# Three moves in a spectral mixture-of-experts kernel: folds on one engine, spectrum columns in halves, the first row list inside the limit search

## The reference, cut to what matters

```
X = np.fft.fft(np.fft.fft(x, axis=1), axis=2).real          # x: 4 x 2496 x 256, float32
x = X.reshape(9984, 256)
# first mixture, 8 experts of 1024 hidden units
logits = x @ w_gate                                          # 9984 x 8
# all (token, expert) pairs in falling order of logit; a token goes to the first expert
# with room left, each expert takes 9984/8 = 1248 tokens
out[assigned to e] = np.maximum(x @ w1[e], 0) @ w2[e]
# second mixture: expert = argmax of its own gate, no capacity
y = softmax_top * sigmoid(x @ w_output_gate)[e] * (relu(x @ w1[e]) @ w2[e])
```

## Time and profile before

| | value |
|---|---|
| median of 3 executions | 1362.06 us |
| the profiled execution: its own time | 1359.75 us |
| its span, first to last instruction | 1358.0 us |
| mean granted TensorE clock | 0.935 |
| PE busy | 1278.2 us (94%) |
| DVE busy | 764.1 us (56%) |
| POOL busy | 571.4 us (42%) |
| ACT busy | 324.8 us (24%) |
| transform: first to last table matmul | 10.81 to 95.6 us |
| features | 95.6 to 133.7 us |
| first five phases | 135.8 to 254.6 us |
| first list | to 289.1 us |
| first product of the first mixture | 298.66 us |

### The profile page before, as it was taken

How to read it: one execution, slowest core, us unless ns; L and a number is a source line. 1 busy time by engine, 2 the same in 40 slices (tenths; PEclk the granted TensorE clock), 3 DMA queues, 4 the chain that set the end, 5 groups by cost and what they waited for, 6 DMA issues and landing times.

```text
span 1358.0 us, 30727 instructions
## 1 busy us (share of the span) xinstructions
PE 1278.2 (94%) x10398; PEld 1176.8 (87%) x10399; DVE 764.1 (56%) x2012; ACT 324.8 (24%) x787; POOL 571.4 (42%) x548
## 2 busy tenths in 40 slices
PE   8999899669999999899999998999999999999996
PEld 5667888548979888889899997999999999999996
DVE  5945888877586678875544544443333443433332
ACT  0013010023222323333332331222222222222221
POOL 5900011225665666565647441612443242544411
PEclk9999555579999999999999998999999999999998
DMA  8707232013212222222222221221232121232110
GB/s 336 253 30 268 100 135 86 2 31 109 85 56 75 65 75 66 68 73 82 62 83 75 73 85 41 81 75 39 78 104 76 39 84 60 77 106 75 47 39 20
DMA packets 63129, 115.98 MB, mean 85 GB/s; under 512 B 7736, under 2 KB 45377, under 8 KB 62912
## 3 DMA queue, kind: packets, MB, share of 16 engines
q1 hardware_dynamic: 39264, 72.16, 15.3%
q0 software_dynamic: 11808, 31.03, 6.9%
q10 hardware_dynamic: 11968, 11.63, 3.0%
HBM read 81.64 MB, written 34.45 MB: 85 GB/s over the span
## 4 chain that ended last, share of the span: by engine, by line
PE 74%; DVE 11%; issue 2%; DMA 1%; ACT 1%; POOL 0%; ACTq 0%; DVEq 0%; POOLq 0%; SPq 0%
PE bank L1123 22%; PE bank L1125 22%; PE bank L1124 21%; PE bank L1004 3%; PE bank L987 3%; DVE hot_r L1784 2%; PE bank L1272 1%; PE bank L1135 1%; DVE hot_q L1785 1%; DVE hot_q L1783 1%; DVE hT_low L1954 1%; DVE arena L1663 1%; DVE xT_low L1947 0%; PE bank L1015 0%; DVE arena L1728 0%
## 5 line engine op out<-in xcount | busy, mean ns | idle before, releaser
L1123 PE MATMUL bank<-weights_high,hT_high 128*128 (+1 forms) x1328 | 388.6, 293 | 0.0
L1125 PE MATMUL bank<-weights_high,hT_low 128*128 (+1 forms) x1328 | 378.4, 285 | 0.0
L1124 PE MATMUL bank<-weights_low,hT_high 128*128 (+1 forms) x1328 | 377.2, 284 | 0.0
L1123 PE MATMUL bank<-xT_high,weights_high 128*128 128x256 f32 (+2 forms) x1072 | 334.8, 312 | 9.2 <-DVE hT_low L1954 3.7
L1125 PE MATMUL bank<-xT_high,weights_low 128*128 128x256 f32 (+2 forms) x1072 | 330.7, 308 | 0.0
L1124 PE MATMUL bank<-xT_low,weights_high 128*128 128x256 f32 (+2 forms) x1072 | 329.8, 308 | 0.0
L1124 PEld LDWEIGHTS bank<-weights_low,hT_high 128*128 128x128 f32 x1328 | 250.4, 189 | 0.0
L1123 PEld LDWEIGHTS bank<-weights_high,hT_high 128*128 128x128 f32 x1328 | 250.2, 188 | 0.1
L1125 PEld LDWEIGHTS bank<-weights_high,hT_low 128*128 128x128 f32 x1328 | 250.2, 188 | 0.0
L1123 PEld LDWEIGHTS bank<-xT_high,weights_high 128*128 128x128 f32 x1072 | 204.2, 190 | 24.2 <-DVE hT_low L1954 7.4
L1125 PEld LDWEIGHTS bank<-xT_high,weights_low 128*128 128x128 f32 x1072 | 203.3, 190 | 11.3
(11 more groups left out here) (264 smaller groups left out, 1460.2 us busy)
## 6 DMA issues: line engine op xcount, KB each, us to landing
arena<-middle ACTq DMA_DIRECT2D x44, 258.0 KB
spectrum<-arena SPq DMA_DIRECT2D x39, 256.0 KB, 2.2
arena<-in_w2a_t SPq DMA_DIRECT2D x8, 1024.0 KB, 4.8
raw<-in_w1a SPq DMA_DIRECT2D x8, 1024.0 KB
raw<-in_w2a SPq DMA_DIRECT2D x8, 1024.0 KB
raw<-in_w1b SPq DMA_DIRECT2D x8, 1024.0 KB
raw<-in_w2b SPq DMA_DIRECT2D x8, 1024.0 KB
arena<-in_x SPq DMA_DIRECT2D x4, 768.0 KB, 4.2
```

Source lines behind the costliest of these rows:

```text
L1123: pe.matmul(out_, a[0], b[0], start=start, stop=False)
L1124: pe.matmul(out_, a[0], b[1], start=False, stop=False)
L1125: return pe.matmul(out_, a[1], b[0], start=False, stop=stop)
```

## The change

It has three parts.

1. **Folds.** POOL's subtractions move to DVE as `odd_fold(n)`. `ODD_AT` gives their places between the joins, `FOLDS_AT` puts the additions one or two joins later, and the warm-up products on PE go from 30 to 24.
2. **Features.** The cosine part and the sine part are no longer summed on PE over 257 columns. PE makes 129 + 8 columns of the cosine part with `feat_c`, and with `feat_s` (now two halves of 129 + 8) the alternating row and the sine part; the matmuls have 274 and 137 columns instead of 273 and 273. ACT copies the cosine half to a new buffer `cosine` (3 slots), DVE adds and subtracts the other half from PSUM (`pairs`), and ACT writes the other 127 columns of both rows as a mirrored copy (`mirrored`). Every step now goes over both engines. Logits are added the same way, three times for many steps at once (`pair_logits`).
3. **Lists.** There are three: slots 0 to 2, slots 3 and 4, slots 5 to 7. The first is made inside phases 3 and 4 (`early_list`, `EARLY_AT`): base, running sum, prefix and positions in rounds 2 and 3 of phase 3 and behind its `accept`, then 2, 3, 3, 3 batches in the rounds of phase 4 and 2 behind its `accept`. The second is made during tiles 0 to 23 of the first mixture (`BASE_AT`, `WIDTHS[1]`), its `tokens` in tile 25. POOL gathers the first four tiles before the last addition to `given` and the last two splits of the first slot's weights, and PE's hidden layer waits for 4 of 8 splits instead of 8.

```diff
-LISTS = ((0, SERIAL), (SERIAL, E))
+COSINES = 3
+EARLY = 3
+LISTS = ((0, EARLY), (EARLY, SERIAL), (SERIAL, E))
-SPIN_START, SPIN_LISTS, SPIN_TURN, SPIN_TABLES, SPIN_BRANCH = 30, 12, 2, 24, 4
+SPIN_START, SPIN_LISTS, SPIN_TURN, SPIN_TABLES, SPIN_BRANCH = 24, 12, 2, 24, 4
+BASE_AT = {0: 1, PLACES_AT: 2}
+TOKENS_AT = {GT - 1: 0, 25: 1, PLACES_AT + 16: 2}
+EARLY_AT = {(4, 0): (0, 1), (4, 1): (2, 3, 4), (4, 2): (5, 6, 7), (4, 3): (8, 9, 10), (4, ROUNDS): (11, 12)}
+WIDTHS = {1: dict(zip((4, 5, 6, 8, 10, 14, 15, 16, 18, 20, 21, 22), (1, 2, 1, 1, 1, 1, 1, 1, 1, 1, 1, 1))),
+          2: dict(zip(range(PLACES_AT + 4, PLACES_AT + 14), (1, 1, 1, 2, 2, 2, 1, 1, 1, 1)))}
-        FOLDS_AT = {1: (2,), 2: (3,), 4: (4,), 5: (5,), 7: (6,), 8: (7,)}
+        FOLDS_AT = {2: (2,), 3: (3,), 5: (4,), 6: (5,), 8: (6,), 9: (7,)}
+        ODD_AT = {0: (1,), 3: (2,), 4: (3,), 6: (4,), 7: (5,), 8: (6,), 9: (7,)}
...
             for n in range(NB + 1):
-                sp.wait_ge(s_out[n % 2], n // 2 + 1)
+                sp.wait_ge(s_out, n + 1)
...
+            for u in range(NST):
+                pool.wait_ge(s_stored[u], 16 * len(range(u, NB, NST)))
+            pool.wait_ge(s_wlast, 16)
+            pool.wait_ge(s_blanked, 16 * (E + 1))
+            pool.wait_ge(m1.row, 1)
+            gathers(range(GT))
             add_given(SERIAL - 1)
             for c in range(c, SPLITS):
                 split(0, 0, c)
             pool.wait_ge(s_gates, E)
             split_gates(0, 0, expert_of(0))
...
+            gathers(range(GT, 2 * GT))
...
-                    pe.wait_ge(s_out[n % 2], n // 2 - 1)
+                    pe.wait_ge(s_paired, n - 3)
...
-                pe.matmul(bk[0:m, 0:RC], a, feat_c[:], start=True, stop=False)
-                pe.matmul(bk[0:m, 0:RC], s, feat_s[:], start=False, stop=True).then_inc(s_f_ps, 1)
+                    at_ = slice(g * P, (g + 1) * P)
+                    pe.matmul(bk[:].rearrange("p (h c) -> p h c", h=2)[:, :, 0:RC], seqB[:, at_], feat_s[:],
+                              start=True, stop=False)
+                    pe.matmul(bk[:, 0:RC], seqA[:, at_], feat_c[:], start=False, stop=True).then_inc(s_f_ps, 1)
...
+            def early_list(ph, r):
+                if (ph, r) == (EARLY, 2):
+                    prefix(bank[6][:, 384:384 + E], 1, s_pre)
+                for b in EARLY_AT.get((ph, r), ()):
+                    scatter(list_at(0), b, b, RING, hot_q, list_width(0), b == 0, b == BATCHES - 1)
...
                         if gi == 0:
-                            pe.wait_ge(m.split, e * SPLITS + SPLITS)
+                            pe.wait_ge(m.split, e * SPLITS + DCH * F // PW)
...
+                act.copy(cosine[:, n % COSINES], bk[:, 0:LC])
+                act.copy(both[:, :, rows_at(n)], bk[:].rearrange("p (h c) -> p h c", h=2)[:, :, LC:RC]).then_inc(s_cosine, 1)
...
+                act.wait_ge(s_paired, n + 1)
...
+                act.copy(store[:, u, :, LC:D], store[:, u, ::-1, P - 1:0:-1]).then_inc(s_out, 1)
...
+            def early_lanes(ph, r):
+                for b in EARLY_AT.get((ph, r), ()):
+                    lanes(b, RING, hot_q, list_width(0))
...
+            def odd_fold(n):
+                b, h = loads[n]
+                u = n % 2
+                c0, c1 = PARTS[h]
+                w = c1 - c0
+                if n:
+                    dve.wait_ge(s_odd, n)
+                dve.tensor_tensor(fdif[:, 0:w], xlow[:, u, 0:w], xmir[:, u, 0:w], ALU.subtract).then_inc(s_g2, 1)
+                dve.wait_ge(s_g2, n + 1)
+                o = odd[:, b, c0:c1]
+                dve.tensor_tensor(o[:, :, 1:P], fdif[:, 0:w, 1:P], fdif[:, 0:w, D - 1:P:-1],
+                                  ALU.subtract).then_inc(s_odd, 1)
...
+                c, t = cosine[:, n % COSINES], feature_bank(n)[:, D:D + LC]
+                dve.tensor_tensor(store[:, g % NST, 0, 0:LC], c, t, ALU.add)
+                dve.tensor_tensor(store[:, g % NST, 1, 0:LC], c, t, ALU.subtract).then_inc(s_paired, 1)
...
+            def early_list(ph, r):
+                if (ph, r) == (EARLY, 2):
+                    slot_base(link, 0)
+                    dve.wait_ge(s_given, EARLY + 1)
+                    running(link)
+                if (ph, r) == (EARLY, 3):
+                    dve.wait_ge(s_pre, 1)
+                    link(dve.tensor_tensor(quota[:], quota[:], bank[6][:, 384:384 + E], ALU.add))
+                    positions(link, 0)
+                if (ph, r) == (EARLY, ROUNDS):
+                    positions(link, 1)
+                for b in EARLY_AT.get((ph, r), ()):
+                    one_hots(link, b, b, RING, hot_q, list_width(0))
...
+                if n in BASE_AT:
+                    if n != PLACES_AT:
+                        dve.wait_ge(s_given, SERIAL + 1)
                     running(link)
-                    slot_base(link, 1)
+                    slot_base(link, BASE_AT[n])
```

More of the change, by code:

```diff
@@ L735, in scatter1, with gathers @@
                                                 bounds_check=E * REG - 1, oob_is_err=False).then_inc(m.sent[gi], 16)
[L737 to L740 removed]
+                def gathers(tiles):
+                    if 0 in tiles:
+                        indices(0, 0)
+                    for t in tiles:
                         if t >= GT:
@@ L1838, in _ @@
                     shut(link, src)
[L1839 to L1849 removed]
+            dve.wait_ge(s_hot_used, BATCHES)
+            rows(link, list_at(0), *LISTS[0])
+            dve.sem_inc(m1.row, 1)
             shut(link, open_log)
             reopen(link)
[L1852 to L1854 removed]
+            slots(link)
             on_limit = Count(dve, s_limit)
```

261 lines of the change are left out of this document (125 added, 136 removed).

## The result

The change made the kernel slower. In six executions of each on one chip the median went from 1362.87 us (1362.03 to 1365.91) to 1369.78 us (1366.80 to 1371.55): ratio 1.0048, 95% interval 1.0033 to 1.0062. The forecast was 1349.2, with a range of 1342 to 1358. In the later groups of runs four executions were in a slow state, at 1756 to 2282 us, and are left out of all medians and ratios. The profiled execution took 1368.87 us (span 1367.1), 9.1 us more than that of before; the sum had expected 12.85 us less.

The account below looks back on a forecast made before the run. Stages have different limits: PE in features and mixture, PE waiting for DVE folds in the transform, DVE in the first list. -5.8 - 6.25 - 9.5 + 8.7 = -12.85 us from 1362.06 gives 1349.2 us, range 1342 to 1358.

Parts of the forecast that it names:

- Part 1, folds: Transform: folds on DVE alone shorten PE's gaps and let it begin earlier; gain 5.8 us.
- Part 2, features: Features: 40 steps of 0.71 us instead of 0.92 save 8.4 us, less 2.15 us of added length; gain 6.25 us.
- which the six slots of `store` absorb: Features: stores need 0.04 us over PE's step, 1.7 us over 39 stores, absorbed; first turned weights about 1 us later.
- Part 3, the early list: Phases 3 and 4: making the first list inside the limits costs 25.95 us instead of 35.5; gain 9.5 us.
- A batch 30 columns wide takes 1.54 us on DVE: Phase 4: price of each list batch, instead of 1.76 us; phase 4 grows by 15.1 us together.
- DVE's own idle time before a mark: Phase 3 rounds: only this, 0.55 and 0.58 us, hides the added list work; phase 3 grows by 4.0 us.
- Part 4, the mixture: First mixture: second list's work and POOL's new order cost 8.7 us, bounds 3 and 20.
- near the low end: Mixture tiles 0 to 3: loss taken as 4.5 us from 3.4 to 7.9, since POOL's splits move away.
- (119.93 - 111.32): Mixture: the other list's work cost PE 8.7 us in 120; from it the 13 batches were priced at 2.5 us.
- DVE overflows in tiles 0 to 25: Rival, chance 0.12: DVE 90% full in the mixture, stretches over; loss 18 to 24 us, time 1359 to 1364.
- terms 2, 3 and 4: Features gain 6.25 us, early list gain 9.5 us, mixture loss 8.7 us.

Follow-up runs that it names:

- a1: The kernel before with only the folds changed; 1356.5 us, ratio 0.9962 to the kernel before.
- b3: The kernel before with folds and features changed, and the four small `last_l` writes issued by POOL instead of SP; 1352.9 us, ratio 0.9929 to the kernel before.
- b4: b3 with the first two turned gate weight loads issued ahead of the waits for the stores; 1352.8 us, ratio 0.9921 to the kernel before.
- b2: The full change with POOL's four weight splits of phases 3 and 4 moved behind the first gathers; 1370.5 us, ratio 1.0059 to the kernel before.
- d2: b4 plus PE's part alone of the second list's 13 scatters, sums unread; 1352.5 us, ratio 0.9941 to the kernel before.
- c3: b4 plus DVE's part alone of the second list's batches, running sum, base and positions, unread; 1362.6 us, ratio 1.0027 to the kernel before.
- a3: The kernel before with only the lists and POOL's order changed; 1372.2 us, ratio 1.0072 to the kernel before.

## Why the prediction was wrong

- **Part 1, folds: right.** 5.5 us by the trace, 5.2 by a1; forecast 5.8.
- **Part 2, features: mis-sized.** The step is right (0.69 us; forecast 0.71), and so is that stores need more than PE. The step that failed is "which the six slots of `store` absorb; the last store and behind it the first turned weights ... come about 1 us later". A store takes 0.77 and not 0.75 us, and SP's four small writes for `last_l`, which the change gathers into one piece of 2.72 us, fall where nothing absorbs them. Together with the order of the loads they cost 3.6 us in phase 0, where 1 was forecast; b3 and b4 recover half. 3.3 us were gained in place of 6.25.
- **Part 3, the early list: mis-sized.** Behind the last round it is as forecast: from that round's step to the first turned tile 13.5 us in place of 41.9, so 28.3 us saved against 28.65. The cost failed: "A batch 30 columns wide takes 1.54 us on DVE", less only "DVE's own idle time before a mark". POOL's splits and additions start behind DVE's comparisons, just where the batches now stand, and the sum has no term for them here. Phases 3 and 4 grew by 24.1 us in place of 19.1, and b2 gives back 3.8 of the 5. About 4 us were gained in place of 9.5.
- **Part 4, the mixture: the largest miss.** 17.9 us in place of 8.7. Tiles 0 to 3 and their start cost 9.6 (forecast 5.2), the batches 6.3 (2.5), the last piece with `tokens` 2.1 (1.0). The failed step is the pricing of this work: 4.5 us for tiles 0 to 3 was taken "near the low end", since POOL's splits move away, where PE then waited 2.63 us for the running sum and 3.96 us for the first emptied bank. The batches rest on "(119.93 - 111.32)". That is a difference of busy time and counts scatters as useful PE work; 13 of them at the 0.32 us of d2 are 4.2 us by an estimate. It was also read beside DVE at 94 of 120 us busy, where here DVE already had its comparisons and the other `tokens`; that this is the rest of the miss is argued, not shown. What the runs show is that DVE's work alone, which nobody reads, costs 11 to 12 us (c3). The rival "DVE overflows in tiles 0 to 25" named this mechanism with 18 to 24 us, and the 17.9 lie at its lower edge; it got a chance of 0.12. Its time, 1359 to 1364, was missed as well, since parts 2 and 3 fell short too.
- **The total.** Relative to the profile of before: -5.1 folds, -3.3 features, -3.9 list, +17.9 mixture, +3.5 behind it, of which 3.3 are spread between executions: +9.1. The forecast's own bounds for part 4 (3 to 20) held. That terms 2, 3 and 4 would all fall short together, each because room was counted as free that was in use, was not weighed.

## What to carry to other kernels

Idle time of an engine is room only if no neighbour uses it: before moving work into it, look what POOL and SP do in exactly those microseconds, and price the moved work with the durations that the trace shows beside them. Price a loss in a stretch by the time between two marks of the program and not by busy time, which counts the added work as useful. Here list work was moved out of an open stretch of 35 us, partly into the limit search and partly into a mixture that is bound by PE but paced by DVE's emptied banks. The kernel came out 10 us slower by it (a3), though DVE was only 71% busy in that part of the mixture before (129.0 of 181.4 us). And look for small reorderings beside the intended change: four writes of some 0.7 us each, gathered in one place, cost part of what the features had gained.
